# Two fused layers after a convolution: layer 2 placed ten units behind layer 1, weights of layer 2 split in quarters

## The reference

```
w = softmax(weight) over 7 taps, one set for each of 8 groups of 24 channels
x = causal convolution along the sequence: sum over k of w[k] * x_pad[s + k]

h = x @ w_in                                  # layer 1, 192 -> 2048
P = a0 + a1*h + a2*h*h + a3*h*h*h
Q = 1 + |b0|*|h| + |b1|*h*h
x = (P / (Q + 1e-6)) @ w_out                  # 2048 -> 192

h = x @ w_in2                                 # layer 2, 192 -> 2048
y = (s * max(h, 0)**2 + b) @ w_out2           # 2048 -> 192
```

## Time and profile before

| | us |
|---|---|
| median of 3 runs | 1308.73 |
| profiled execution | 1309.7 |
| its span, first to last instruction | 1307.9 |
| PE busy | 1276.3 (98%) |
| DVE busy | 1138.5 (87%) |
| ACT busy | 1115.1 (85%) |
| POOL busy | 331.7 (25%) |

### The profile page before, as it was taken

The page is one execution under the profiler, slowest core; times in us unless marked ns, Lnnn a source line. Parts: engine busy times, 40 slices in busy tenths (PEclk is TensorE's granted clock), DMA queues, the critical chain, the costliest instruction groups (busy, mean ns, idle before and its releaser), DMA issues.

```text
span 1307.9 us, 16349 instructions
## 1 busy us (share of the span) xinstructions
PE 1276.3 (98%) x5984; PEld 1077.7 (82%) x5984; DVE 1138.5 (87%) x1048; ACT 1115.1 (85%) x1072; POOL 331.7 (25%) x147
## 2 busy tenths in 40 slices
PE   5897999999999999999999999999999999999998
PEld 3665888888888888888888888888888888888887
DVE  5998889998999989998899989999899998979830
ACT  5887898888889888889888888998888898888843
POOL 4333222222222222222222222222222222222210
PEclk8998999999999999999999999999999999999999
DMA  5211000010000100001000010001000000000000
GB/s 137 106 33 25 1 1 13 1 37 1 12 0 0 36 0 12 0 0 36 0 12 0 13 23 0 12 0 36 0 12 0 0 12 1 13 1 13 1 13 13
DMA packets 14045, 20.40 MB, mean 16 GB/s; under 512 B 1472, under 2 KB 9664, under 8 KB 13504
## 3 DMA queue, kind: packets, MB, share of 16 engines
q1 hardware_dynamic: 13872, 20.00, 5.4%
q10 hardware_dynamic: 144, 0.01, 0.0%
HBM read 13.72 MB, written 6.29 MB: 15 GB/s over the span
## 4 chain that ended last, share of the span: by engine, by line
PE 90%; DVE 5%; ACT 2%; issue 2%; POOL 1%; DMA 0%; DVEq 0%; SPq 0%; ACTq 0%
PE o L363 25%; PE h L337 9%; PE h L338 9%; PE h L340 9%; PE h L341 9%; PE h L339 9%; PE o_tail L352 4%; PE o L350 4%; PE o_tail L354 4%; PE o L351 4%; PE o L353 4%; DVE work L737 1%; DVE work L704 1%; DVE work L706 1%; DVE work L739 1%
## 5 line engine op out<-in xcount | busy, mean ns | idle before, releaser
L320 POOL TENSOR_TENSOR gl<-work,gh 128x1024 fp32r<-128x1024 f32 x128 | 307.0, 2398 | 896.2 <-ACT gh L566 896.2
L363 PE MATMUL o<-v,work 128*128 128x192 f32 x2048 | 353.3, 326 | 0.0
L363 PEld LDWEIGHTS o<-v,work 128*128 128x128 f32 x2048 | 339.2, 190 | 10.1
L704 DVE SCALAR_TENSOR_TENSOR work<-work,coef,h 128x1024 f32<-128x1024 f32 x128 | 163.7, 1279 | 91.9 <-ACT work L539 91.9
L337 PE MATMUL h<-x_hi,w_hi 128*128 128x512 f32 x512 | 224.4, 438 | 17.6 <-DVE work L709 13.4
L341 PE MATMUL h<-x_tail,w_tail_lo 128*128 128x512 f32 x512 | 205.0, 400 | 0.0
L338 PE MATMUL h<-x_lo,w_hi 128*128 128x512 f32 x512 | 204.6, 400 | 0.0
L340 PE MATMUL h<-x_tail,w_tail_hi 128*128 128x512 f32 x512 | 204.6, 400 | 0.0
L339 PE MATMUL h<-x_hi,w_lo 128*128 128x512 f32 x512 | 204.2, 399 | 0.0
L537 ACT ACTIVATE work<-h,coef 128x1024 f32<-128x1024 f32 x128 | 154.2, 1205 | 27.8 <-PE h L341 21.4
L569 ACT ACTIVATE work<-work 128x1024 f32<-128x1024 f32 x128 | 135.7, 1060 | 42.4 <-DVE work L704 38.8
(11 more groups left out here) (78 smaller groups left out, 1544.8 us busy)
## 6 DMA issues: line engine op xcount, KB each, us to landing
out_dram<-y_out SPq DMA_DIRECT2D x16, 384.0 KB, 2.6
xt<-in_x_main_dram SPq DMA_DIRECT2D x7, 518.0 KB, 4.5
xt_tail<-in_x_tail_dram SPq DMA_DIRECT2D x8, 259.0 KB, 5.1
work<-in_moe_w_out_dram SPq DMA_DIRECT2D x1, 1536.0 KB, 9.7
v<-in_moe_w_out_dram SPq DMA_DIRECT2D x1, 1536.0 KB, 6.3
work<-in_moe_w_in_dram SPq DMA_DIRECT2D x1, 1024.0 KB, 8.4
work<-in_moe_w_in_dram SPq DMA_DIRECT2D x2, 512.0 KB, 5.8
xt<-in_x_main_dram SPq DMA_DIRECT2D x2, 259.0 KB, 6.4
```

The source lines that it names most:

```text
L320: nc.gpsimd.tensor_tensor(gl[:, j % 2, :], r_buf[j % 2], gh[:, j % 2, :].bitcast(F32), ALU.subtract).then_inc(gl_ready, 1)
L363: last = pe.matmul(o2[:, c // 2, c % 2, 0:D], g, v2[:, f, :], start=(f == 0 and c % 2 == 0), stop=(f == FT - 1), skip_group_check=True)
L704: nc.vector.scalar_tensor_tensor(q_buf[buf], w_abs, b0_abs, h_flat, ALU.add, ALU.mult).then_inc(z_done, 1)
```

## The change

SKEW becomes 10 and OUT1_LAG 2. On PE the second product of layer 1 moves to the end of an iteration, behind both products of layer 2, and does all high parts (gh) before the low parts (gl). Layer 2's first product is ordered by parts of x (high, low, tail), with separate waits in a tile's first unit. The x2 split moves on DVE ahead of z of j = 2, on ACT ahead of t. The weights of layer 2 are loaded and split in quarters: four casts of 1024 columns in ACT's iterations 3 to 6, eight low parts of 512 columns on POOL in iterations 4 to 11. The seven tail diagonals get a buffer of their own and are made at the end of ACT's iterations 6 to 9; PE's tail taps move from iterations 9 and 10 to 8 and 9. The vector engine's taps are spread anew.

```
-    SKEW = 11
-    OUT1_LAG = 3
+    SKEW = 10
+    OUT1_LAG = 2
...
-    X2_STEP = OUT1_LAG - 1
+    X2_STEP = OUT1_LAG
...
-               9: (("tail", (0, 1, 2)),), 10: (("tail", (3, 4, 5, 6)),)}
+               7: (("pair_b", (3, 4, 5, 6)),), 8: (("tail", (0, 1, 2)),), 9: (("tail", (3, 4, 5, 6)),)}
...
+        tail_diag = [work2[:, 2, k * P:(k + 1) * P] for k in range(TAPS)]
...
+        W2_HIGH_AT = {3: ("tail", 0), 4: ("main", 0), 5: ("main", 1), 6: ("tail", 1)}
+        W2_LOW_AT = {4: ("tail", 0, 0), 5: ("tail", 0, 1), 6: ("main", 0, 0), 7: ("main", 0, 1),
+                     8: ("main", 1, 0), 9: ("main", 1, 1), 10: ("tail", 1, 0), 11: ("tail", 1, 1)}
+        TAIL_DIAG_AT = {6: (0,), 7: (1, 2), 8: (3, 4), 9: (5, 6)}
...
+            def second_product_1(n, k, buf):
+                pe.wait_ge(gh_ready, counted(n - OUT1_LAG + 1))
...
+                pe.wait_ge(gl_ready, counted(n - OUT1_LAG + 1))
...
+                    if unit(n - OUT1_LAG) and not tile(t) and j == OUT1_LAG - 1:
+                        second_product_of_layer_1(n, j, t)
                     if tile(t):
                         second_product_of_layer_2(t, j, m, k2)
...
                     if unit(m):
                         if k2 == 0:
-                            for ready in (x2_hi_ready, x2_lo_ready, x2_tail_hi_ready, x2_tail_lo_ready):
-                                pe.wait_ge(ready, counted(t2 + 1))
-                            pe.wait_ge(w_hi_ready, 10)
+                            pe.wait_ge(w_hi_ready, 12)
                             pe.wait_ge(w_lo_ready, 12)
...
+                        first_product_of_layer_2(k2, x2p, t2)
                     if not tile(t):
                         second_product_of_layer_2(t, j, m, k2)
+                    if unit(n - OUT1_LAG) and (tile(t) or j != OUT1_LAG - 1):
+                        second_product_of_layer_1(n, j, t)
...
+                    for k in TAIL_DIAG_AT.get(n, ()) if isinstance(n, int) else ():
+
+                        act.wait_ge(w_lo_ready, 10)
+                        diagonal(k, 1)
...
+                    if j == X2_STEP and tile(t - 1):
+                        split_o1(t, hi, lo)
+                        sum_o1_tail(t)
+                        split_o1_tail(t, tail)
                     h_flat = h2_flat if in_h2(n) else h1_flat
                     if unit(n):
                         dve.wait_ge(t_ready, counted(n + 1))
```

More of the change, by code:

```diff
@@ L353, in second_product_1 @@
-                    pe.matmul(o1[:, :], v1_hi[:, f, :], gl[:, buf, c], start=False, stop=final)
-                    last = pe.matmul(o1_tail[:, :], tail, gl[:, buf, c], start=False, stop=final)
-                last.then_inc(out1_done, 1)
+                    pe.matmul(o1_tail[:, :], tail, gh[:, buf, c], start=(f == 0), stop=False)
+                pe.wait_ge(gl_ready, counted(n - OUT1_LAG + 1))
+                for half in range(2):
+                    f = 2 * k + half
+                    c = slice(half * TOK, (half + 1) * TOK)
+                    tail = v1_tail[:, f].rearrange("p a b -> p (a b)")
+                    pe.matmul(o1[:, :], v1_hi[:, f, :], gl[:, buf, c], start=False, stop=(f == FT - 1))
+                    last = pe.matmul(o1_tail[:, :], tail, gl[:, buf, c], start=False, stop=(f == FT - 1))
@@ L366, in second_product_2, with conv_taps @@
                 last.then_inc(out2_done, 1)
-            def conv_taps(bank, rows, taps, first, last):
+            def conv_taps(bank, rows, taps, first, last, diagonals=diag):
                 for k in taps:
-                    done = pe.matmul(conv_bank[bank], diag[k], rows[:, k:k + TOK], start=(k == first),
+                    done = pe.matmul(conv_bank[bank], diagonals[k], rows[:, k:k + TOK], start=(k == first),
                                      stop=(k == last))
@@ L438, in phase @@
                     early = isinstance(n, int) and n < SKEW
-                    if unit(n) and not early:
+                    if unit(n) and not (isinstance(n, int) and n <= SKEW):
                         product_of_layer_1(n, j, t, parity)
@@ L545, in phase @@
                         copy_of_conv(conv[:, 1, :], 1)
-                    if first(t) and j == 7:
+                    if first(t) and j == 6:
                         act.wait_ge(conv_summed, 3)
@@ L551, in phase @@
                         act.wait_ge(conv_summed, 4)
-                        for k in range(TAPS):
-                            diagonal(k, 1)
                         act.wait_ge(x1_lo_ready, 4)
                         copy_of_conv(conv[:, 1, :], 0)
-                    if second(t) and j == 3:
+                    if second(t) and j == 2:
                         act.wait_ge(conv_summed, 5)
                         copy_of_conv(conv_tail[:, :], 1)
-                    if j == X2_STEP and tile(t - 1):
-                        act.wait_ge(out1_done, counted(t * UNITS))
-                        act.wait_ge(x2_tail_lo_ready, counted(t - 1))
-                        nc.scalar.copy(x2_sum, o1_tail[TAIL:P, :]).then_inc(x2_tmp_ready, 1)
                     if unit(n - 2):
```

148 lines of the change are left out of this document (88 added, 60 removed).

## The result

The changed kernel takes 1326.14 us (median of 4 runs, 1324.48 to 1326.87) beside 1309.03 for the kernel before (4 runs, 1307.24 to 1309.42): ratio 1.0137, 95% interval 1.0124 to 1.0149, so it is slower by 17 us. Its profiled execution took 1326.87 us, its span is 1325.1, 17.2 more than before.

What follows compares the result with a forecast made beforehand. PE bounds the kernel with an unbroken matmul queue after the start. Loop 12.6, start 2.0 and drain 3.6 make 18.2; 1309.7 + 18.2 = 1327.9, less 1 for the median: 1327 us; own range 1319 to 1335, stated range 1314 to 1336.

Steps and rivals of the forecast that it cites:

- loop: Tiles 2 to 15: late z delays PE by 0.9 us a tile, 12.6 us in all, between 6 and 20.
- start: Before PE's queue is unbroken: 2.8 - 1.7 + 0.9 = +2 us, between -3 and +6.
- drain: At the end PE waits 2.6 us for gh and 1.0 for gl of unit 127: +3.6 us.
- The chain: Loop, j = 2: x2 split makes z 1.05 us late, so t3, the square and layer 2's second product slip; 0.9 us a tile.
- Rival A: Loop: slack before layer 2's second product is over 1 us, so the loop costs nothing; 1314.4 us, chance 0.14.
- rival B: Loop: each of 14 pairs of gaps brings a stretch at 1.2 GHz, at 1.7 us; 1351 us, chance 0.06.
- The walk of z: Start: z stepped from unit 3 at 47.51 to unit 9 at 96.7, 4.1 us earlier than before; unit 10 at 120.4.
- the 0.9 us counted for the lower clock: Start: half of the 1.7 us lost today after 124.38 was counted again, for gaps of about 1 us.
- Rival C: Start: all diagonals ready by about 91 us, no wait, unit 11's product at 111.2; 1312.5 us, chance 0.07.
- The wait for gh: Drain: PE waits 2.6 us for gh of unit 127, or 1.4 in all if r1 took some 2 us less.
- The stall of r1: Drain: r1 of unit 127, started 0.07 us behind a POOL instruction, again takes 3.38 us by the shared port rule.
- The edits costed at nothing: Loop: the other edits cost 0; ordering matmuls by parts of x was bounded at 0.05 us a unit, 6 us either way.

Runs made afterwards that it cites:

- the two experiments that take one of them away each: Changed kernel with layer 2's second product behind its first except in a tile's first unit: 1316.95 us; with the x2 split shortened in odd tiles 3 to 13: 1321.09 us.
- The run with r1 alone: Changed kernel, but POOL's gl of unit 126 waits until DVE's r1 of unit 127 is through: 1324.72 us, ratio 1.0128.

## Why the prediction was right, point by point

1326.14 us were measured, 1327 forecast, and the three causes are the three that it named. Their sizes were 11.1 instead of 12.6 (loop), 1.25 instead of 2.0 (start) and 4.8 instead of 3.6 (drain); the errors cancel in part, so it is partly luck that the sum came within 1 us.

- Loop. The chain held step by step: z 5.90 us behind the product, the next first product 0.1 late, the square's end at 12.56 (forecast 12.55), the second product at 12.71 (forecast 12.8). A tile loses 0.8 us and not 0.9. That the lateness of z and the missing slack are needed together was argued, and is shown by the two experiments that take one of them away each. Rival A (the loop absorbs it) is out by the 14 waits, rival B by the clock of 1.00.
- Start. The walk of z was right to about 1 us (72.33 and 95.85 for 72.9 and 96.7; 120.38 for 120.4), the wait is 13.32 for 13.6, the product of unit 11 at 124.97 for 124.8. The term that was wrong is the 0.9 us counted for the lower clock behind that product: the window from 120 shows 1.00. Two errors cancel ahead of it: PE resumed at 101.13 and not at 102.05, and the lower clock behind the stop cost some 2.7 us (4.50 instead of 2.65 for the three taps, 1.17 instead of 0.34 for the matmul behind them, both against the run with early diagonals) and not 1.7. Rival C's condition was not met, but its price was about right: it put the time at 1312.5, and the run with early diagonals took 1313.88. The clock did fall there, against C's words: the window from 100 to 110 shows 0.83 behind the wait of 2.54.
- Drain. The step that failed is that PE reaches unit 126's second product as early as today's blocks allow, 16.9 us after unit 127's first product. It ended at about 17.8: a wait of 0.74 for layer 2's ReLU stood ahead of it, which the prediction did not see. The wait for gh shrank by about as much, to 1.44 for 2.6, and that for gl was 0.81 for 1.0. Not seen either was the wait of 0.79 for x_tail: the prediction followed PE's delay into the second product alone, and not through ACT's list, where the copy for x2 stands behind a ReLU that needs a product made late. The four waits sum to 3.8; with a weight load of 0.22 exposed at each, an estimate from the earlier trace rows, 4.7.
- The stall of r1. It returned (3.39 us, started 0.07 us behind POOL's gl). That agrees with the Trainium skill (SBUF — State Buffer, Who interferes with whom), by which the engine that issues first blocks the other. The run with r1 alone shows the other direction, 3.41 us for gl behind g.
- The edits costed at nothing. The order by parts is shown to cost nothing. That casts and low parts in quarters cost nothing is only seen, in that no wait of PE in the loop or behind unit 11 hangs on them.

That the loop's term came near is partly luck too. The prediction read the earlier trace rows as a PE that never waits. But in the kernel before a first product is late once a tile, because t3 comes late behind the x2 split; PE and DVE's t3 there:

```profile
202.37 0.39 PE L341 MATMUL h<-x_tail,w_tail_lo 128*128 128x512 f32 x1
202.71 0.50 PE L337 MATMUL h<-x_hi,w_hi 128*128 128x512 f32 x1
...
201.37 1.28 DVE L709 SCALAR_TENSOR_TENSOR work<-work,coef,h 128x1024 f32<-128x1024 f32 x1
```

The step is 0.34 us instead of 0.23, and that iteration lasts 0.2 us longer than the others. In the changed kernel the gaps that the prediction named cost 0.69 us in an even tile and 0.86 in an odd one, 10.9 in all. Off go the 0.2 us a tile that were there before, 2.9; on top come the seven stops for gl, 1.9, and the longer iterations, 1.2. The prediction counted none of these three.

## What to carry to other kernels

When PE is the bound and its queue is unbroken, a reordering is judged by the slack of each operand at its new place: write down when the operand is complete and when it is read, for the one iteration in which a helper step stands ahead of it, and not for the mean iteration. A wait for a set of small preparations (here two diagonals of 0.68 us) makes the engine that waits stand until the iteration is done in whose list the last one stands. A busy share of 100% does not show that nothing waits: the short stops of this loop, before and after, are seen in the distances between the starts of matmuls. A delay at the end of a program is to be followed through every in-order list that it enters; here moving one block of independent work in between was worth more (3.4 us in the trace) than speeding up the stalled instruction (1.2).

## What the runs showed of the hardware

- A POOL subtraction and a DVE instruction with two SBUF operands delay each other in both directions, and the one that started second, by 0.07 and 0.11 us, is the one that takes longer: 3.39 instead of 1.22 us for DVE, 3.41 instead of 2.38 for POOL.
- Gaps of 0.3 to 0.4 us on PE once every 77.6 us left the granted clock at 1.00 here; after the stop of 13.3 us six tap records took 5.49 us instead of 2.74, and the first product at 108.86 was at the full clock again (its next half follows 1.17 us later).
- Small diagonals issued together on ACT cost 0.68 us for two and 1.27 for four, about 0.3 each.
